# Signalling with the last sum in place of draining TensorE's queue

## The reference

```
attn_out = attention(q_l, k_l, v_l, q_g, k_g, v_g)   # local window 32 and 32 global tokens
x = attn_out as [4, 544, 512]
# the mix
x_prev = x shifted by one token
xk = mu_k * x + (1 - mu_k) * x_prev
xr = mu_r * x + (1 - mu_r) * x_prev
k = maximum(xk @ w_k, 0)            # 512 -> 1024, "keys"
v = (k * k) @ w_v                   # 1024 -> 512, "values"
r = sigmoid(xr @ w_r)               # 512 -> 512, "receptance"
x = r * v
# routing: each token picks one of 8 experts, by the largest logit or the expert of the token before
out[token] = p[e] * (maximum(x @ w1[e], 0) @ w2[e])
```

## Time and profile before

| | |
|---|---|
| median of 3 runs | 657.29 us (656.52 to 658.33) |
| the profiled execution's own time | 656.79 us |
| its span in the profile | 655.1 us |
| TensorE busy | 615.8 us, 94% of the span |
| TensorE weight loads busy | 509.0 us, 78% |
| VectorE busy | 417.8 us, 64% |
| ScalarE busy | 307.6 us, 47% |
| GpSimd busy | 168.5 us, 26% |
| mean granted TensorE clock | 0.979 of full speed |

### The profile page before, as it was taken

How to read it: one execution, slowest core, us unless ns; L and a number is a source line. 1 busy time by engine, 2 the same in 40 slices (tenths; PEclk the granted TensorE clock), 3 DMA queues, 4 the chain that set the end, 5 groups by cost and what they waited for, 6 DMA issues and landing times.

```text
span 655.1 us, 14914 instructions
## 1 busy us (share of the span) xinstructions
PE 615.8 (94%) x4468; PEld 509.0 (78%) x4469; DVE 417.8 (64%) x1148; ACT 307.6 (47%) x678; POOL 168.5 (26%) x241
## 2 busy tenths in 40 slices
PE   7999999999999999999999159999999999999995
PEld 6888888877787887789797047878888888888883
DVE  3777779466987878778797869485272273263531
ACT  4767779486146326506437006374251262162621
POOL 4554556400000000000000016555242153143140
PEclk9999999999999999999999669999999999999999
DMA  9978882020300000010043343578172063054000
GB/s 336 328 263 292 283 279 104 2 81 1 113 17 0 33 33 0 16 50 0 17 162 144 142 159 125 199 276 302 32 242 92 32 241 105 32 186 152 11 27 3
DMA packets 31636, 80.41 MB, mean 123 GB/s; under 512 B 4330, under 2 KB 7146, under 8 KB 31600
## 3 DMA queue, kind: packets, MB, share of 16 engines
q1 hardware_dynamic: 25520, 65.81, 28.4%
q0 software_dynamic: 3200, 8.92, 4.0%
q10 hardware_dynamic: 2880, 5.24, 2.3%
HBM read 71.83 MB, written 9.70 MB: 124 GB/s over the span
## 4 chain that ended last, share of the span: by engine, by line
PE 86%; DVE 8%; ACT 2%; issue 2%; POOL 1%; DVEq 0%; ACTq 0%; POOLq 0%
PE banks L755 22%; PE banks L757 22%; PE banks L756 22%; PE banks L631 3%; PE banks L889 3%; PE banks L698 2%; PE banks L707 2%; DVE banks L1093 2%; PE banks L661 2%; PE banks L645 1%; PE banks L858 1%; PE banks L675 1%; PE banks L671 1%; PE banks L722 1%; PE banks L737 1%
## 5 line engine op out<-in xcount | busy, mean ns | idle before, releaser
L1093 DVE CUSTOM_DVE_ANT_0 banks<-x,xT 128x512 f32<-128x512 f32 x136 | 91.3, 718 | 0.4 <-DMA xT<-in_w 0.2
L1363 DVE TENSOR_SCALAR hid<-banks 128x512 f32<-128x512 f32 x40 | 27.6, 691 | 89.6 <-PE banks L757 88.1
L1390 ACT ACTIVATE prob<-neg,negmax 128x160 f32<-128x160 f32 (+1 forms) x136 | 59.1, 436 | 29.6 <-DVE negmax L948 19.9
L755 PE MATMUL banks<-we_hi,hid_hi 128*128 x160 | 67.1, 419 | 1.9 <-DVE hid_lo L1368 1.9
L755 PE MATMUL banks<-we_hi,xg_hi 128*128 x160 | 65.1, 407 | 0.6 <-DVE xg_lo L1344 0.6
L1493 ACT ACTIVATE k_sum<-banks 128x512 f32<-128x512 f32 (+2 forms) x40 | 21.4, 534 | 94.0 <-PE banks L757 89.5
L756 PE MATMUL banks<-we_lo,hid_hi 128*128 x160 | 63.3, 395 | 0.0
L757 PE MATMUL banks<-we_hi,xg_lo 128*128 x160 | 63.2, 395 | 0.0
L756 PE MATMUL banks<-we_lo,xg_hi 128*128 x160 | 63.2, 395 | 0.0
L757 PE MATMUL banks<-we_hi,hid_lo 128*128 x160 | 63.2, 395 | 0.0
L555 POOL MEMSET xg<- 128x1024 f32 x1 | 1.0, 952 | 238.0 <-PE banks L757 238.0
(11 more groups left out here) (223 smaller groups left out, 1409.7 us busy)
## 6 DMA issues: line engine op xcount, KB each, us to landing
we_raw<-in_w_e SPq DMA_DIRECT2D x56, 512.0 KB, 4.9
qk<-in_qk_t SPq DMA_DIRECT2D x32, 448.0 KB, 5.7
vw<-in_v_t SPq DMA_DIRECT2D x32, 256.0 KB, 5.3
w_raw<-in_w_mix ACTq DMA_DIRECT2D x20, 256.0 KB, 3.8
x_rows<-x SPq DMA_DIRECT2D x17, 256.0 KB, 2.0
xT<-in_w SPq DMA_DIRECT2D x8, 256.0 KB, 3.3
xT<-in_w_e SPq DMA_DIRECT2D x4, 512.0 KB, 5.9
first_raw_end<-in_w_e SPq DMA_DIRECT2D x4, 512.0 KB, 3.5
```

Source lines behind the costliest of these rows:

```text
L755: pe.matmul(dst, left[0], right[0], start=first, stop=False)
L1093: dve.tensor_tensor_reduce(product[:, k % 2, :], x2[:, t, :], w9(e), 1.0, 0.0, ALU.mult, ALU.add, dot[:, t % 2, e:e + 1]).then_inc(dotted, 1)
L1363: dve.tensor_scalar(hid[:, D * h:D * (h + 1)], ps_h[:, h, :], 0.0, None, ALU.max).then_inc(hid_ready, 1)
L1390: act.activation(prob[:, t % 2, c], neg[:, c], ACT.Exp, scale=-1.0, bias=negmax[:, t % 2, k:k + 1], accum_out=rsum[:, t % 2, k:k + 1]).the ...
```

## The change

The two `drain` instructions of each group and the two `mix_used` semaphores are taken out. Who waited for `mix_used[0]` at group g now waits until all 8 x g key slices are summed (`k_summed`), and who waited for `mix_used[1]` until all tiles of the groups before are summed (`r_summed`). Both counters are counted up by the last matmul of a sum, as before. No other instruction is added or moved.

```
-        mix_used = [sem("mix_used_k"), sem("mix_used_r")]
...
@@ SyncE
-                    sp.wait_ge(mix_used[0], GROUPS)
+                    sp.wait_ge(k_summed, FC * GROUPS)
...
@@ TensorE
                     pe.wait_ge(k_copied, FC * g + f + 1)
                     keys_part(g, tiles, f)
-                pe.drain().then_inc(mix_used[0], 1)
...
                     mm.then_inc(r_summed, 1)
-                pe.drain().then_inc(mix_used[1], 1)
...
@@ VectorE
-                    dve.wait_ge(mix_used[1], GROUPS)
+                    dve.wait_ge(r_summed, NT)
                     first_weights(range(0, PARTS // 2))
...
@@ ScalarE
                     if c == 1 and not (isinstance(g, int) and g == 0):
-                        act.wait_ge(mix_used[m], g)
+                        act.wait_ge(*((r_summed, first_tile(g)) if m else (k_summed, FC * g)))
...
                 if not tiles_after:
-                    act.wait_ge(mix_used[0], GROUPS)
+                    act.wait_ge(k_summed, FC * GROUPS)
                     rounded_weights(0, slice(0, 1), range(0, 3))
```

## The result

| | before | after |
|---|---|---|
| median | 656.9 us (4 runs, 656.4 to 658.33) | 652.49 us (4 runs, 652.11 to 653.23) |
| profiled execution | 656.79 us, span 655.1 | 652.11 us, span 650.4 |
| PE busy | 615.8 us | 613.2 us |

The ratio is 0.9931, with a 95% interval of 0.9912 to 0.9949: faster by 4.4 us. The forecast was 652.9: a gain of 4.37 us, taken from 657.29, the median of three runs that was known then. With a fourth run the median before is 656.9, so the gain came out as forecast and the time 0.4 us lower.

What follows compares the result with a forecast made beforehand. TensorE, 86% of the chain that ended last, was taken as the bound. Group 0 gives 0, group 1 1.03, groups 2 to 4 3.34: 4.37 us off 657.29 gives 652.9 us, range 651.3 to 655.3.

Steps and rivals of the forecast that it cites:

- The pause is the drain's and is worth some 0.56 us each: TensorE's extra time behind keys and receptance comes from the drains, not the change of stage: 5.61 us for all ten.
- Rival C: At the drains only the last matmul's tail goes, 0.16 us each, 1.3 us for eight: 656.0 us; 8 in 100.
- Group 0 yields nothing: At group 0's third value tile TensorE waits 1.09 us longer for VectorE's product, whose chain does not move: 0 gained.
- Group 1 loses 0.15 us: At group 1's third value tile the margin to VectorE's product shrinks to 0.05 us; 0.15 charged, 1.03 us gained.
- Rival D: Group 1's third value tile waits for VectorE's product, so the group yields nothing: 654.1 us; 8 in 100.
- Groups 2 to 4 yield all of theirs: In the last three groups the drains' whole cost is saved: 1.21 + 1.11 + 1.02 = 3.34 us.
- The moved waits cost nothing: ScalarE, VectorE and SyncE waiting on the sums' counters instead of drain signals: 0, at most 0.1 us either way.
- rival E: Ahead of the experts the clock returns later, all 36 transposes at half clock, 2.3 us added: 654.9 us; 8 in 100.
- F: The clock stays at half into the first expert's matmuls, so the kernel is slower: 659.4 us at 13 us; 4 in 100.

Runs made afterwards that it cites:

- the seventeen drains: The changed kernel with 17 drains put into group 3 alone, behind its key slices, receptance tiles and half value tiles: 659.69 us, ratio 1.0036.
- the version with the early product: The changed kernel with VectorE's first product of a group put ahead of the last two steps of the next group's mixed inputs: 650.83 us, ratio 0.9909.

## Why the prediction was right

*The pause is the drain's and is worth some 0.56 us each.* Right. With the drains put back 656.46 to 656.87 us, without them 652.5, and no gap above an ordinary step was left at the boundaries of 512-column stages (at the two narrower ones some 0.03 us of slow steps stayed). Rival C, the matmul's tail only, would have given 656.0, and was out by the seventeen drains too. What it leaves out is what stands in the rows: the drain record ends 0.43 us behind the last matmul's start where a step is 0.23; then the next instructions are issued, up to 0.31 us; then the weights of the first matmuls are not loaded ahead. The Trainium skill (TensorE: Matmul & The Clock Gate, Single matmul latency) gives 166 ns as the fixed part of a lone matmul, by which a drain would cost 0.17 us, an estimate. That is less than half of the least that any of the 37 drains of three of these traces took (0.38), so the trace does not bear it out as the price of a drain.

*Group 0 yields nothing.* Right, by a run of its own (656.57 us with its two drains out) and by the wait that grew to 1.25 us. Its cause, the chain that begins behind the table load, is shown by the run that moved the load.

*Group 1 loses 0.15 us.* The trace shows 0.11, all of it in slow steps: the margin was 0.06 us where 0.05 had been worked out. Rival D, in which the product does not follow, did not come: the product ended 0.92 us earlier (222.36 in place of 223.28), 0.65 of it inside the group.

*Groups 2 to 4 yield all of theirs.* Right but for the slow steps at the two narrower boundaries. From first key matmul to first key matmul (in group 4 to the first product) the two traces differ by 0.02, 1.07, 1.21, 1.07 and 0.98 us in groups 0 to 4, where 0, 1.03, 1.21, 1.11 and 1.02 had been forecast. Groups 2 to 4 gave 3.26 of 3.34 us, and the whole mix 4.35 of 4.37, since group 1 gave a little more. In group 4 VectorE's idle time fell by 0.45 us, about what the second drain had held TensorE back, and did not reach zero.

*The moved waits cost nothing.* Right within what was measured, with one small term missed: the signal on a drain was itself part of the pause, 0.04 us. It did not falsify the sum, since the sum was made from gaps that held it.

*The clock.* Rivals E and F did not come. The transposes grew by 0.35 us and the wait for the gathered rows covered that. Both rivals tied the clock's return to the shift of 4.4 us, and the traces don't: it moved by 3.1 us between two profiles of one kernel. In the one with the latest return, 4.80 us, the transposes took 6.46 us and left no wait for the rows, and the rest of the span was no longer than in the others; what a still later return costs, no run shows. Two readings of the prediction were a little off. The page shows the two slices of the routing at six tenths, not at 66%. And a transpose follows the one before after 0.213 us at half clock and 0.109 at full, so that rival E's worst case adds some 2.0 us ahead of the wait and not 2.3.

Two things stay open. Why the 0.06 us between a drain's end and the next matmul grow to 0.17 where a second wait and a change of stage come together is read from where the wait's record lies, and was not tried by taking that wait away; nor was the 0.03 us at a drain behind a matmul with a signal. And the 1.8 us that the version with the early product is under the change can't be told, by the runs, from the 1.5 expected. Its trace shows 1.6 us in group 0 and 0.14 in group 1: the 1.5 counted how late group 0's third tile starts (1.41) and left out the slow steps behind that wait.

## What to carry to other kernels

Read the price of a drain from the starts of the matmuls on both sides, over some ten of them, and compare with a boundary that has none; its own record, here up to 4.3 us, says nothing. Then ask for each one what the engine meets next: a pause ahead of a wait on another engine's chain is free, and its removal only lengthens that wait, unless the chain itself begins behind the pause. Where the completion count of a last matmul says the same as the drain, use the count, and look in the waiting engine's idle stretches for the piece that the freed engine now waits on.

## What had not been expected of the hardware

A drain of TensorE is not one price: counted over the 12 matmuls behind it, it takes 0.38 to 0.41 us where at most one wait follows (14 of the 17), 0.44 to 0.51 where two waits follow, about 0.6 at the end of the keys in the hardware loop, where register instructions stand behind it as well, and 0.04 us more when it counts up a semaphore itself. Its record ends 0.03 us later where the matmul ahead of it counts one up.
